# Attention and two MLP blocks on one core: the hand-written order of calls on four engines, rearranged around two change-overs

## What is computed

```python
attn = softmax(where(same_cluster, q @ k.T / 8, -1e9)) @ v      # x: 1536 tokens x 512
h = x @ w_in                                                    # 512 -> 2048
g = where(h >= 1, h, where(h <= -1, 0, (h + 1) ** 2 / 4))
x = g @ w_out                                                   # 2048 -> 512
xn = x / sqrt(mean(x * x) + 1e-6) * rms_g
y = (silu(xn @ w_gate) * (xn @ w_val)) @ w_out2                 # 512 -> 1536 -> 512
```

## Time and profile before

| what | value |
|---|---|
| median of 3 runs | 847.98 us (845.19 to 849.59) |
| the profiled execution's own time | 846.89 us |
| its span in the trace | 845.1 us |
| PE, DVE, ACT, POOL busy | 95%, 78%, 58%, 47% of the span |
| attention | 0 to about 285 us |
| first MLP | 285 to about 542 us |
| second MLP | 542 to 845 us |

### The profile page before, as it was taken

How to read it: one execution, slowest core, us unless ns; L and a number is a source line. 1 busy time by engine, 2 the same in 40 slices (tenths; PEclk the granted TensorE clock), 3 DMA queues, 4 the chain that set the end, 5 groups by cost and what they waited for, 6 DMA issues and landing times.

```text
span 845.1 us, 15305 instructions
## 1 busy us (share of the span) xinstructions
PE 804.9 (95%) x5341; PEld 731.6 (87%) x5341; DVE 657.3 (78%) x1220; ACT 493.8 (58%) x895; POOL 400.4 (47%) x356
## 2 busy tenths in 40 slices
PE   4899999999999989999999999889999999999998
PEld 4798898898888879989899888779999999999997
DVE  4798898898898697665665668997877787878666
ACT  3788887887887667665555558838623222222221
POOL 0133533344467960760560562893296381929000
PEclk9999999999999999999999999999999999999999
DMA  6866546645542100010110010210020201101012
GB/s 136 187 156 145 126 107 144 133 107 128 135 94 61 33 13 26 26 50 26 26 51 27 26 50 26 63 38 1 27 63 1 76 1 51 39 19 33 28 44 80
DMA packets 65507, 54.92 MB, mean 65 GB/s; under 512 B 30112, under 2 KB 52640, under 8 KB 65440
## 3 DMA queue, kind: packets, MB, share of 16 engines
q1 hardware_dynamic: 65440, 54.06, 25.6%
HBM read 27.30 MB, written 3.15 MB: 36 GB/s over the span
## 4 chain that ended last, share of the span: by engine, by line
PE 73%; DVE 12%; issue 7%; ACT 5%; POOL 2%; DMA 1%; DVEq 0%; SPq 0%; ACTq 0%; POOLq 0%
PE ps L744 31%; PE ps L766 12%; PE ps L778 11%; PE ps L628 5%; PE ps L612 4%; PE ps L585 4%; PE ps L588 3%; DVE ptl L1296 2%; DVE sf L1287 2%; DVE gl L1434 1%; PE ps L656 1%; ACT pbuf L855 1%; PE ps L657 1%; DVE tl L1462 1%; DVE tl L1276 1%
## 5 line engine op out<-in xcount | busy, mean ns | idle before, releaser
L744 PE MATMUL ps<-th,wh 128*128 128x256 f32 x840 | 240.3, 286 | 7.0 <-DVE pair L1386 2.8
L744 PE MATMUL ps<-tl,wh 128*128 128x256 f32 x840 | 238.3, 284 | 0.0
L744 PE MATMUL ps<-th,wl 128*128 128x256 f32 x840 | 238.3, 284 | 0.0
L744 PEld LDWEIGHTS ps<-th,wh 128*128 128x128 f32 x840 | 161.6, 192 | 12.5 <-DVE tl L1276 2.5
L744 PEld LDWEIGHTS ps<-tl,wh 128*128 128x128 f32 x840 | 161.7, 192 | 2.0
L744 PEld LDWEIGHTS ps<-th,wl 128*128 128x128 f32 x840 | 161.6, 192 | 0.0
L1287 DVE TENSOR_SCALAR_CACHE_REDUCE sf<-ps 128x768 f32<-128x768 f32 x96 | 91.2, 950 | 26.3 <-PE ps L588 25.5
L1808 POOL TENSOR_TENSOR wl<-wraw,wh 128x448 fp32r<-128x448 f32 x80 | 105.5, 1347 | 1.4
L845 ACT ACTIVATE pth<-ps 128x512 fp32r<-128x512 f32 x144 | 84.4, 589 | 29.4 <-PE ps L612 17.4
L855 ACT ACTIVATE pbuf<-sf,minn 128x768 f32<-128x768 f32 x96 | 89.6, 934 | 19.8 <-DVE sf L1287 19.6
L1296 DVE TENSOR_TENSOR ptl<-ps,pth 128x512 fp32r<-128x512 f32 x144 | 95.4, 681 | 3.9 <-ACT pth L845 3.8
(11 more groups left out here) (138 smaller groups left out, 1792.9 us busy)
## 6 DMA issues: line engine op xcount, KB each, us to landing
q<-atile SPq DMA_DIRECT2D x32, 192.0 KB, 3.3
k<-atile SPq DMA_DIRECT2D x32, 192.0 KB, 3.6
o1raw<-in_moe_w_out SPq DMA_DIRECT2D x8, 512.0 KB, 3.7
nat<-in_q SPq DMA_DIRECT2D x16, 192.0 KB, 3.8
nat<-in_k SPq DMA_DIRECT2D x16, 192.0 KB, 4.0
...
```

Of the source, the lines that this page charges most:

```text
L744: last = pe.matmul(dst[:, 0:HC], a[w][:, j, kt, :], b[c][:, j, kt, :], start=(opened and kt == 0 and i == 0), stop=(kt == KH - 1 and i == ...
```

## The change

Only the order of calls changes, on DVE, ACT, POOL and SP: around steps 0 to 6 (from attention to the first MLP) and around steps 18 to 33 (between the MLPs). No call is added or dropped and no wait is edited. Where a loop over `step(s)` ends earlier, its calls are written out. The core of the diff (the other lines are of the same kind):

```diff
@@ -532,11 +532,11 @@
             load_up(9)
             load_up(10)
             load_out2(8)
-            load_out2(12)
             load_out2(9)
             load_out2(10)
+            load_out2(13)
+            load_out2(12)
             load_out2(11)
-            load_out2(13)
...
@@ -1054,36 +1054,37 @@
                     for m in range(KT):
                         take_y(s - 1, m)
 
+            second_t_hi(4, 1)
             snap(0)
-            second_t_hi(4, 2)
             copy_corner(0)
+            second_t_hi(5, 1)
             bend(0, 0)
+            second_t_hi(6, 1)
             snap(1)
+            hidden_hi(0, 0)
             bend(0, 1)
-            hidden_hi(0, 0)
+            second_t_hi(7, 2)
+            hidden_hi(0, 1)
+            bend(1, 0)
             copy_corner(1)
...
             copy_corner(23)
-            scale_x(1, 0, 1)
             bend(23, 0)
             scale_x(1, 1, 1)
-            squares(1, 2, 2)
-            scale_x(1, 2, 2)
+            squares(1, 2, 1)
             hidden_hi(23, 0)
-            t_hi(4, 0, 1)
             inverse_out(0)
-            t_hi(4, 1, 1)
+            scale_x(1, 2, 1)
             snap(24)
             bend(23, 1)
+            copy_corner(24)
             hidden_hi(23, 1)
+            squares(1, 3, 1)
+            scale_x(1, 3, 1)
             sums_hi(1)
-            t_hi(4, 2, 1)
...
@@ -1509,78 +1519,82 @@
             first_sum(0)
             second_sum(0)
             inner_first(0)
+            second_t_lo(4, 1)
             inner_second(0)
-            second_t_lo(4, 1)
             second_half(0)
             first_half(0)
+            second_t_lo(5, 1)
+            maximum(0, 0)
             first_sum(1)
-            maximum(0, 0)
             second_sum(1)
+            inner_first(1)
+            hidden_lo(0, 0)
+            inner_second(1)
             maximum(0, 1)
-            hidden_lo(0, 0)
-            inner_first(1)
-            inner_second(1)
             second_half(1)
-            second_t_lo(5, 1)
+            second_t_lo(6, 1)
             hidden_lo(0, 1)
-            second_t_lo(6, 2)
+            second_t_lo(7, 1)
+            maximum(1, 0)
+            second_t_lo(8, 1)
...
+            t_lo(3, 0, 1)
             inner_second(22)
             second_half(22)
+            first_half(22)
+            hidden_lo(21, 1)
+            t_lo(3, 1, 2)
             sums_lo(0)
-            hidden_lo(21, 1)
             maximum(22, 0)
+            t_lo(3, 3, 1)
             take_y(21, 0)
-            first_half(22)
             take_y(21, 1)
-            take_y(21, 2)
             maximum(22, 1)
             first_sum(23)
+            hidden_lo(22, 0)
+            take_y(21, 3)
+            second_sum(23)
+            inner_first(23)
+            t_lo(3, 4, 1)
+            take_y(21, 2)
+            inner_second(23)
+            hidden_lo(22, 1)
+            second_half(23)
+            t_lo(3, 5, 1)
+            first_half(23)
+            inverse(0)
             add_squares(1, 0)
-            hidden_lo(22, 0)
-            second_sum(23)
-            take_y(21, 3)
-            inner_first(23)
-            inner_second(23)
-            inverse(0)
-            second_half(23)
-            t_lo(3, 2, 1)
-            hidden_lo(22, 1)
-            t_lo(3, 3, 1)
-            first_half(23)
-            t_lo(3, 4, 2)
...
             second_sum(24)
             inner_first(24)
             inner_second(24)
             maximum(23, 1)
-            t_lo(4, 0, 1)
             second_half(24)
             hidden_lo(23, 1)
+            add_squares(1, 2)
+            take_y(23, 0)
+            scale_gate(24)
             first_half(24)
-            scale_gate(24)
+            take_y(23, 1)
             sums_lo(1)
-            t_lo(4, 1, 2)
             take_y(23, 2)
             product(24)
             first_sum(25)
             second_sum(25)
-            take_y(23, 1)
-            take_y(23, 0)
             hidden_lo(24, 0)
             inner_first(25)
+            take_y(23, 3)
+            add_squares(2, 0)
             inner_second(25)
-            take_y(23, 3)
             second_half(25)
+            scale_gate(25)
             first_half(25)
-            scale_gate(25)
+            t_lo(4, 0, 1)
             product(25)
             first_sum(26)
             second_sum(26)
+            hidden_lo(25, 0)
             inner_first(26)
-            hidden_lo(25, 0)
-            t_lo(4, 3, 1)
-            inverse(1)
+            t_lo(4, 1, 1)
             inner_second(26)
             second_half(26)
+            scale_gate(26)
             first_half(26)
-            scale_gate(26)
-            t_lo(4, 4, 2)
-            add_squares(2, 0)
+            inverse(1)
+            t_lo(4, 2, 3)
+            add_squares(2, 1)
+            t_lo(4, 5, 1)
+            product(26)
             first_sum(27)
-            product(26)
             t_lo(4, 6, 1)
             second_sum(27)
-            add_squares(2, 1)
+            add_squares(2, 2)
             hidden_lo(26, 0)
-            add_squares(2, 2)
             inner_first(27)
+            sums_lo(2)
             inner_second(27)
-            sums_lo(2)
...
+            high_out(7)
             sum_up(8)
+            low_out(7, 0)
+            low_out(7, 1)
             high_up(8)
-            low_up(8, 0, 1)
-            fill_out(7)
-            low_up(8, 1, 3)
...
             low_up(9, 0, 3)
-            t_sum(4, 0, 1)
             sum_up(10)
             low_up(9, 3, 1)
             high_out(8)
             high_up(10)
-            low_up(10, 0, 2)
+            high_out(9)
+            low_up(10, 0, 1)
+            t_sum(4, 0, 1)
+            low_up(10, 1, 1)
             low_out(8, 0)
+            t_sum(4, 1, 1)
             low_up(10, 2, 2)
-            high_out(9)
-            t_sum(4, 1, 1)
-            high_out(10)
             low_out(9, 0)
```

More of the change, by code:

```diff
@@ L1081, in _ @@
             bend(2, 1)
-            take_y(1, 3)
-            t_hi(2, 4, 2)
+            t_hi(2, 2, 2)
+            copy_corner(3)
             hidden_hi(2, 1)
-            t_hi(2, 6, 1)
-            copy_corner(3)
+            t_hi(2, 4, 3)
             bend(3, 0)
@@ L1141, in _ @@
             snap(22)
             bend(21, 1)
-            t_hi(3, 3, 2)
+            hidden_hi(21, 0)
+            sums_hi(0)
             hidden_hi(21, 1)
+            copy_corner(22)
+            t_hi(3, 2, 2)
             bend(22, 0)
-            copy_corner(22)
+            bend(22, 1)
+            take_sums(0)
+            hidden_hi(22, 0)
+            t_hi(3, 4, 1)
+            snap(23)
             t_hi(3, 5, 1)
             squares(1, 0, 1)
-            bend(22, 1)
-            take_sums(0)
@@ L1178, in _ @@
+            t_hi(4, 1, 1)
+            squares(2, 1, 1)
             copy_corner(25)
-            squares(2, 1, 1)
             silu(25)
             take_sums(1)
+            squares(2, 2, 1)
+            t_hi(4, 2, 2)
+            snap(26)
+            hidden_hi(25, 0)
             t_hi(4, 4, 1)
-            snap(26)
-            scale_x(2, 0, 1)
-            hidden_hi(25, 0)
-            rms(1)
             scale_x(2, 1, 1)
@@ L1562, in _ @@
             maximum(3, 1)
+            first_half(4)
             hidden_lo(3, 1)
-            first_half(4)
+            take_y(3, 0)
             maximum(4, 0)
+            maximum(4, 1)
+            take_y(3, 1)
+            first_sum(5)
             hidden_lo(4, 0)
-            take_y(3, 0)
-            first_sum(5)
-            take_y(3, 1)
             second_sum(5)
             inner_first(5)
-            maximum(4, 1)
             inner_second(5)
@@ L1592, in _ @@
             take_y(5, 1)
-            for s in range(7, 19):
+            for s in range(7, 18):
                 step(s)
+            first_sum(18)
+            second_sum(18)
+            inner_first(18)
+            inner_second(18)
+            second_half(18)
+            first_half(18)
+            maximum(18, 0)
+            maximum(18, 1)
+            hidden_lo(18, 0)
+            hidden_lo(18, 1)
+            take_y(17, 0)
             first_sum(19)
+            take_y(17, 1)
+            second_sum(19)
             take_y(17, 2)
-            second_sum(19)
-            take_y(17, 3)
             inner_first(19)
@@ L1602, in _ @@
             first_half(19)
+            take_y(17, 3)
             maximum(19, 0)
-            hidden_lo(19, 0)
             maximum(19, 1)
             first_sum(20)
+            hidden_lo(19, 0)
             second_sum(20)
@@ L1610, in _ @@
             second_half(20)
+            hidden_lo(19, 1)
             first_half(20)
-            hidden_lo(19, 1)
+            take_y(19, 1)
+            take_y(19, 0)
+            take_y(19, 3)
             maximum(20, 0)
-            take_y(19, 0)
-            take_y(19, 1)
+            first_sum(21)
+            maximum(20, 1)
             take_y(19, 2)
-            maximum(20, 1)
-            take_y(19, 3)
+            second_sum(21)
```

(26 more changed lines are left out.)

181 lines of the change are left out of this document (89 added, 92 removed).

## The result

The changed kernel takes 838.13 us (median of 4 runs, 837.71 to 839.54), the kernel before in the same comparison 848.79 (4 runs, 845.19 to 849.91): ratio 0.9885, 95% interval 0.9852 to 0.9918, so 1.15% faster. The forecast was 841.5 in a range of 836.5 to 848.5; the sign and the range held, the gain was larger. The profiled execution took 838.31 with a span of 836.5, against 846.89 before: 8.58 us, where the sum had 5.6.

The account below looks back on a forecast made before the run. DVE was taken as the bound in 532 to 570, with a slow clock behind a long wait. Terms 0.9 + 5.9 - 2.0 + 0.8 = 5.6 us, from 846.89 to 841.3, forecast as 841.5, range 836.5 to 848.5.

Parts of the forecast that it names:

- the first change-over: From attention to the first MLP: earlier DVE calls gain 0.8 us, most lost again; between -0.5 and 3.3.
- the full stretch: DVE from 532 to `hidden_lo(24, 0)`: calls moved out let `down(24)` start 5.9 us earlier; bounds 2.8 and 6.7.
- payback: Between `hidden_lo(24, 0)` and j5 of `up(27)`: three more `t_lo(4, ...)` cost 2.0 us; upper bound 4.4.
- `o1`'s stretch: POOL at q7, ahead of `down(19)`: splitting `o1` first gains 0.7 idle and about 0.2 restart, 0.9 us.
- at nothing: Moves put at no gain or loss: SP's loads, POOL's `t_sum(4, 0)`, ACT's steps 20 to 29, steps 3 to 6 and 29 to 33.
- the slow clock: Behind the 1.98 us wait in `up(24)`: clock 0.50 for 3.4 us costs 1.4 us; none expected after the change.
- Chunk 1's three calls: Three `t_lo` moved out of DVE's full stretch to behind `hidden_lo(24, 0)`: 1.65 and two in 2.65 us.
- Chunk 0's two: Two `t_lo` of 1.45 and 1.64 us moved to the front of DVE's full stretch, where DVE waited for ACT.
- `add_squares(1, 0)`: Moved within DVE's full stretch from where POOL was idle to where POOL works: a cost of 0.8 us.
- The wait for `z`: TensorE's wait for ACT's `inverse_out(0)` in `up(24)`: expected 1.0 us in place of 1.98.
- Rival 2: POOL's work runs on beside DVE's calls between `hidden_lo(24, 0)` and `up(27)`, stretching them: slower, 852.3, chance 0.11.
- Rivals 1 and 3: 1: put-off calls due before DVE catches up, 848.1, chance 0.23; 3: all DVE relief reaches TensorE, 834.6, chance 0.06.

Follow-up runs that it names:

- e7_tlo4: The changed kernel with chunk 1's three `t_lo` back ahead of `hidden_lo(24, 0)` on DVE, their `t_hi` moved ahead on ACT; 845.49 us, ratio 0.9981.
- e5_o1: The changed kernel with POOL's order around q7 and q8 put back as before the change; 839.55 us, ratio 0.9914.
- e6_again: The changed kernel run once more, nothing altered; 839.6 us (5 runs), ratio 0.991 to before.
- e1_first: The kernel before with only the change's new order of steps 0 to 6 on ACT, DVE and POOL; 844.33 us, ratio 0.9971.
- e2_second: The kernel before with only the change's new order from step 18 on, with SP's; 840.48 us, ratio 0.9926.

## Why the prediction was right, and where it was off

As a whole the sum was 3.0 us short of the profiled gain (5.6 against 8.57), and it came so near because errors of both signs met: 2.4 too little for the first change-over, 2.25 too little for the full stretch, 0.9 too much payback and 0.2 too little for `o1`'s stretch, against 2.65 lost late that it had at nothing.

**What bounds it.** Right: DVE in 532 to 570, and the slow clock behind a long wait. e7_tlo4 shows both most plainly.

**POOL's `o1`, 0.9.** Right: 0.91 by e5_o1. The stretch around it gave up to 1.42, since `down(20)`'s wait for `hidden_lo(20, ...)`, 0.42 in step 21 of before, went as well; it stands in no term of the sum.

**DVE's full stretch, 5.9.** The mechanism is right, the size near: 8.15 in the profiled pair, 6.64 in the repeated execution. `hidden_lo(24, 0)` ended 9.9 us earlier against the start of step 20 (69.69 before, 59.81 after; 61.46 in e6_again), where I had 6 to 7. The parts were sized wrong in both directions. Chunk 1's three calls were put at 4.30; they are worth 6.0, since a wait of that length also brings the slow clock. Chunk 0's two were put at 3.09 and are worth 0.9: TensorE lost 1.9 in step 23 and got 1.1 back in step 24. `add_squares(1, 0)`, charged 0.8 for running beside POOL, ran while POOL stood idle for its load:

```profile
536.79 0.74 POOL L1813 TENSOR_TENSOR wraw<-corner,wraw 128x256 f32<-128x256 f32 x1 [2.52 <-DMA wraw<-in_moe_w_val]
```

**The wait for `z` and the slow clock.** Both are gone, better than the 1.0 us I left. But e1_first, with before's order there, shows neither in its profile, so that order doesn't always have them. That the new order rules them out isn't shown; in its twelve profiled executions neither came in `up(24)`.

**The payback, 2.0.** Mis-sized: 1.08 and 0.87 in 26 to 30. And the three `t_lo(4, ...)` that I charged don't pay it, as e7_tlo4 has it unchanged. It comes from the change from step 18 on (e2_second has it, e1_first hasn't), for the most part as a gap of 0.28 us at j2 of `up(27)` and one of 0.55, from 0.19 before, at `down(27)`. Which moved call makes them wasn't tried: this cause stays open.

**The first change-over, 0.8.** The term that failed most: 3.18. The step was "DVE must do all of `second_t_lo`, `maximum(1, 0)` and `first_half(1)` before `first_sum(2)` in either order". That counts work and not when it can start. DVE stood idle 2.32 us for `snap(1)` and 0.61 more; the new order puts a `second_t_lo` and `maximum(0, 0)` there, `hidden_lo(0, 0)` came 1.9 us earlier and `first_sum(2)` 3.1. I had taken only TensorE's waits from this stretch, and not DVE's own. What was feared as lost again at j6 was 0.77 us. The 3.18 includes 0.63 at `up(7)`, which waited in before and not after.

**"At nothing".** Wrong for ACT in steps 29 to 33: TensorE hardly waited there, but the moved `take_y` and `snap` gave up the cover that had kept it so, and 2.65 us were lost in the profiled execution, and in the four others in which POOL came first at `scale_gate(31)`.

**The rivals.** Rival 2's place didn't come about: POOL stood idle from 565.6 us on, and four of the last five `t_lo(4, ...)` took 0.68. Its mechanism, POOL beside DVE, is real and sharper than I had it, as e7_tlo4's calls at 1.6 us show. Rivals 1 and 3 didn't come: the three terms of gain were at or over their values (12.4 us together), and the payback and the late waits took 3.7 of that.
